# Recurrence kernel: the fourth level of an inverse in one piece, and two pieces of filling work swapped

## The chip, the cores and the metric

The kernel runs on one core of a Trainium2 chip. The metric is the device time in microseconds of one execution. A profiled execution has a span as well, from its first instruction to its last.

## What is computed

Three parts follow one another. The first is a recurrence over 768 steps for 4 x 8 heads, each with a 40 x 40 state:

```
y[t]  = r[t] . state
Sa    = state . a[t]
state = state * w[t] - outer(Sa, b[t]) + outer(v[t], k[t])
```

The second part is a mixture of four attention experts over the heads' outputs (scores, softmax, top 2 of 4), the third a gated MLP with a mixing over the sequence. The change touches the first part alone, which takes about the first half of the time.

## The kernel before, in words

The recurrence is computed in blocks of 128 steps. One block of one batch entry, with all its 8 heads, is a *unit*; there are 4 x 6 = 24. A unit has 4 chunks of 32 steps, 0 to 3. Within a chunk the steps depend on one another through a lower triangular matrix n; its inverse T is built by doubling, in five *levels*, numbered i = 0 to 4 (`level`, line 752): each multiplies a power of n by itself and by the product so far. So the "second level" is i = 1, the "fourth" i = 3 and the "fifth" i = 4. A level works on 8 blocks and issues 16 matmuls, 2 for each block; the profile counts each as two, so a whole level is 32 weight loads and 32 matmuls, two of its blocks 8 of each. After a level VectorE turns the new power (line 1059) and adds the product (line 1094, semaphore `q_added`), and ScalarE spreads the turned power over two masked copies (line 541, `spread`) and copies the power as a right operand (`copy_power`, `power_copied`; it shows as "ACT pq L533"). The next level waits for both.

The state goes from chunk to chunk through a chain of three *hops* on TensorE (`hop`, line 923) with VectorE in between (`chain`, line 1138):

- hop 0: akz times the values (line 941, needs no state) and a_ch times state_z (line 947) give g; VectorE copies it (line 1145).
- hop 1: tz times g (line 957); VectorE makes the values vu_tok in two instructions (line 1153).
- hop 2: keys times values (line 969), the state's products; VectorE adds them to the state (state_sum, line 1161) and spreads the decayed sum as state_z (line 1173), for which hop 0 of the next chunk waits.

The order of all work is written out by hand. On each engine a loop over u calls, after every hop (c, j) of chunk c, a function `between(u, c, j)` with filling work for other units (TensorE's is at line 846). Its unit numbers are t = u + 2, v = u + 1, w = u - 1 and x = u - 2. What stands in `between(u, c, 1)` runs while VectorE makes the values of the chunk, and ahead of hop 2; what stands in `between(u, c, 2)` runs behind the state's products, while VectorE makes state_sum and state_z. TensorE executes in this order, so a wait in front of filling work holds the next hop too.

Filling work that matters here, of TensorE: first Gram products of t (line 718); `turn_states(w)` (line 701) and `turn_outputs(u - 3)` (line 806), transposes of earlier states and outputs into PSUM, read by ScalarE in `states_read` (line 555, tile state_n) and `outputs_taken` (line 594, tile y_raw); `from_values` (line 842), which adds the part of the outputs that comes from the values; `turn_values` (line 696), which waits for state_n; and the levels of unit v, all on line 768. Levels 1 to 4 and the turned outputs use the same PSUM bank, 3, so level 1 waits until y_raw is taken (`y_taken`). ScalarE's order in a unit begins with the two spreads of tz, then states_read, then outputs_taken. In the last two units TensorE also has matmuls that fold two weight matrices (line 747).

Of the kernel before, what the change touches and what calls it, by code (L numbers as in the profile page):

```python
# [25 lines left out]
def recurrence(nc, z, loads, weights, x_out, shared):  # L26
# [17 lines left out]
    N8 = 2 * NC  # L44
# [7 lines left out]
    with ExitStack() as ctx:  # L52
# [11 lines left out]
        def at(u, s, c=None):  # L64

            return u * per[s] + (per[s] if c is None else c)
# [97 lines left out]
        kb_read = sem("kb_read", 2)  # L164
# [9 lines left out]
        vu_read = sem("vu_read", 2)  # L174
# [54 lines left out]
        def valid(u):  # L229
            return 0 <= u < UNITS  # L230
# [300 lines left out]
        def _(act):  # L531
            def copy(dst, src):
                return act.activation(dst, src, ACT.Copy)  # L533

            def spread_power(u, i):

                act.wait_ge(turned[i], at(u, turned[i]))
                if u > 0:
                    act.wait_ge(level_ready[i], at(u - 1, level_ready[i]))
                for j in range(2):  # L540
                    act.activation(powers_z[:, i, :, j, :], powers[:, i, :, :], ACT.Copy, scale=parity[:, j:j + 1])\  # L541
                        .then_inc(spread[i], 1)
# [51 lines left out]
            def outputs_taken(w):  # L594

                act.wait_ge(y_turned, at(w, y_turned))
                if w > 0:
                    act.wait_ge(y_done, at(w - 1, y_done))
                copy(y_raw[0:CHANNELS, :], bank[Y_TURN_BANK][0:CHANNELS, :]).then_inc(y_taken, 1)
# [51 lines left out]
            for u in range(UNITS + 3):  # L651
                r, t, v, w, x = u + 3, u + 2, u + 1, u - 1, u - 2
                if valid(u):
                    spread_t(u)
                if u == 0:
                    copy_power(1, 0)
                    spread_power(1, 1)
                if valid(w):
                    states_read(w)
                if valid(u - 3):  # L660
                    outputs_taken(u - 3)
                if u == 0:
                    pad_a(2)
                if valid(t):
                    spread_power(t, 0)
                if valid(v):
                    spread_power(v, 2)
                    copy_power(v, 1)
                if valid(w):
                    values_read(w)  # L670
                if valid(x):
                    outputs_copied(x)
                if valid(v):
                    spread_power(v, 3)
                    copy_power(v, 2)
                if u == UNITS - 1:
                    folded(0)
                if u == UNITS:
                    folded(2)
                if valid(r):  # L680
                    pad_a(r)
                if valid(v):
                    spread_power(v, 4)
                    keys_read(v)
                if valid(t):
                    copy_power(t, 0)
                    spread_power(t, 1)
                if u == UNITS - 1:
                    folded(1)
                if u == UNITS:  # L690
                    folded(3)

        @block.tensor
        def _(pe):
# [78 lines left out]
            def turn_states(w):  # L773

                pe.wait_ge(state_done, at(w, state_done, NC - 1))
                for c in range(NC):
                    for b in range(2):
                        col = (c % 2 * 2 + b) * P
                        ins = turn_channels(bank[TURN_BANKS[c // 2]][:, col:col + P],
                                            state[:, w % 2, c, b].rearrange("p a d -> p (a d)"))  # L780
                ins.then_inc(state_turned, 1)
# [19 lines left out]
            def turn_outputs(w):  # L801

                pe.wait_ge(y_copied, at(w, y_copied))
                for c in range(NC):
                    src = y_tok[:, c, :, :].rearrange("p x d -> p (x d)")
                    ins = pe.transpose(bank[Y_TURN_BANK][0:CHANNELS, c * P:c * P + P], src[:, 0:CHANNELS], ident[:, :])
                ins.then_inc(y_turned, 1)
# [27 lines left out]
            def from_values(w, first):  # L835

                for c in range(first, first + 2):
                    for x in range(2):
                        for q in range(Q):
                            a, p, g, blk = place(c, q)  # L840
                            col = c * X + x * D
                            pe.matmul(bank[Y_BANK][rows32(g), col:col + D], rvu[rows64(p), c * 2 + x, 1 - a, :],
                                      kb_tok[rows64(p), w % 3, a, c, x, :], start=False, stop=(c < 2),
                                      skip_group_check=True)

            def between(u, c, j):


                t, v, w, x = u + 2, u + 1, u - 1, u - 2
                if (c, j) == ((0, 0) if u > 0 else (0, 2)) and valid(t):  # L850
                    first_grams(t)
                if (c, j) == (0, 0):
                    if valid(w):
                        if valid(v - 1):
                            pe.wait_ge(kb_read, at(v - 1, kb_read))
                        else:
                            pe.wait_ge(vu_read, at(w - 1, vu_read))
                        turn_states(w)
                    if valid(u - 3):

                        if valid(u):
                            pe.wait_ge(q_added[4], at(u, q_added[4]))
                        else:
                            pe.wait_ge(oi_read, 2)
                            pe.wait_ge(y_taken, at(u - 4, y_taken))
                        turn_outputs(u - 3)
                if (c, j) == (0, 1):
                    if valid(x):
                        from_values(x, 2)
                    if valid(v):  # L870
                        if valid(u - 3):
                            pe.wait_ge(y_taken, at(u - 3, y_taken))
                        level(v, 1, 0, 2)
                if (c, j) == (0, 2) and valid(v):
                    level(v, 1, 2, N8)
                if (c, j) == (1, 0):
                    if valid(w):
                        pe.wait_ge(state_n_read, at(w, state_n_read))
                        turn_values(w)
                    if valid(x):  # L880
                        from_states(x, 2)
                if (c, j) == (1, 1):
                    if valid(t):
                        level(t, 0, 0, 4)
                    if valid(v):
                        level(v, 2, 0, 2)
                if (c, j) == (1, 2) and valid(v):
                    level(v, 2, 2, N8)
                if (c, j) == (2, 0):
                    if valid(t):  # L890
                        grams(t, 1)
                    if valid(w):
                        if valid(x):
                            pe.wait_ge(y_copied, at(x, y_copied))
                        r_products(w)
                if (c, j) == (2, 1):
                    if valid(t):
                        pe.wait_ge(akz_read, at(t, akz_read))
                        level(t, 0, 4, N8)
                    if valid(v):  # L900
                        level(v, 3, 0, 2)
                if (c, j) == (2, 2) and valid(v):
                    level(v, 3, 2, N8)
                if (c, j) == (3, 0):
                    if valid(v):
                        if valid(w):
                            pe.wait_ge(vu_read, at(w, vu_read))
                        turn_keys(v)
                    if valid(w):
                        pe.wait_ge(rvu_read, at(w, rvu_read))  # L910
                        pe.wait_ge(state_n_read, at(w, state_n_read))
                        from_states(w, 0)
                if (c, j) == (3, 1):
                    if valid(w):
                        from_values(w, 0)
                    if valid(v):
                        level(v, 4, 0, 2)
                if (c, j) == (3, 2) and valid(v):
                    level(v, 4, 2, N8)
                for f in range(folds_upto(u, c, j) - folds_after.get((u, c, j), 0), folds_upto(u, c, j)):  # L920
                    fold(f)
# [1056 lines left out]
```

## Time and profile before

| | us |
|---|---|
| median of 3 runs | 989.86 |
| lowest and highest | 985.64, 992.79 |
| the profiled execution | 986.91 |
| its span | 985.0 |
| TensorE busy (share of the span) | 937.3 (95%) |
| TensorE weight loads busy | 676.4 (69%) |
| VectorE busy | 490.3 (50%) |
| ScalarE busy | 447.5 (45%) |

Busy time of an engine is the union of its instructions' times. TensorE appears twice, as PE (matmuls) and PEld (weight loads), which overlap; matmuls are pipelined, so starts of successive weight loads tell more of its pace than durations do. "Idle before <- X" is the idle time of the engine just ahead of an instruction and what ended it; "issue" is a wait for nothing that the profile shows.

### The profile page before, as it was taken

Reading aid. Unit: us, or ns where it says so; the run is one execution under the profiler, and the core shown is the slowest. Engines: PE = TensorE matmul, PEld = TensorE weight load, DVE = VectorE, ACT = ScalarE, POOL = GpSimd, SP = SyncE. Lnnn points to the kernel's source line nnn. Section 1 sums busy time; section 2 is a strip of 40 time slices with the busy share of each in tenths; the row PEclk is TensorE's granted clock in tenths of the full one; section 3 lists DMA queues with packets and bytes.
Section 4 is the critical chain, followed back from the end, with each engine's and each line's share of the span. In section 5 each row is a group of like instructions: output and inputs, shape, how many; then the busy total and the mean of one; then the engine's idle time right before and its main releaser. Section 6 shows DMA issues by size and latency. Waiting matters only on the chain.

```text
span 985.0 us, 36043 instructions
## 1 busy us (share of the span) xinstructions
PE 937.3 (95%) x15444; PEld 676.4 (69%) x15444; DVE 490.3 (50%) x1395; ACT 447.5 (45%) x1074; POOL 266.2 (27%) x442
## 2 busy tenths in 40 slices
PE   6899999999999999999998999999999999999998
PEld 4788888888888888886655655566555665556555
DVE  7687777677677777754155244321444214342120
ACT  6455655555555555553237234342343423434501
POOL 7444545445445545522300001100011000110021
PEclk8799999999999999999999999999999999999999
DMA  4234333335333333241160000001000000000001
GB/s 153 71 108 115 111 100 105 100 93 152 101 99 106 100 94 112 68 122 31 51 217 1 2 0 1 1 28 54 0 1 2 27 14 0 1 2 27 14 0 41
DMA packets 37455, 59.68 MB, mean 61 GB/s; under 512 B 9136, under 2 KB 24304, under 8 KB 37296
## 3 DMA queue, kind: packets, MB, share of 16 engines
q1 hardware_dynamic: 37296, 57.37, 19.6%
q8 instruction: 123, 2.02, 0.9%
q14 instruction: 36, 0.29, 0.1%
HBM read 49.49 MB, written 7.86 MB: 58 GB/s over the span
## 4 chain that ended last, share of the span: by engine, by line
PE 80%; DVE 8%; issue 6%; ACT 5%; DMA 1%; POOL 0%; DVEq 0%; ACTq 0%; POOLq 0%
PE banks L1640 13%; PE banks L768 8%; PE banks L1579 5%; PE banks L1557 5%; PE banks L1591 4%; PE banks L1531 4%; PE banks L1608 4%; PE banks L1621 4%; PE banks L701 4%; PE banks L1652 4%; PE banks L947 3%; PE banks L829 3%; PE banks L969 3%; PE banks L696 2%; DVE state_z L1173 2%
## 5 line engine op out<-in xcount | busy, mean ns | idle before, releaser
L541 ACT ACTIVATE powers_z<-powers,parity 128x256 f32<-128x256 f32 x240 | 108.5, 500 | 162.3 <-DVE powers L1059 162.1
L1428 POOL TENSOR_TENSOR v_st<-v_st,u_t 128x384 f32<-128x384 f32 x32 | 31.9, 997 | 450.5 <-DVE v_st L1795 450.5
L768 PE MATMUL banks<-pq,powers_z 64*64 64x64 f32 (+1 forms) x3072 | 132.1, 225 | 18.4 <-ACT pq L533 13.6
L1640 PE MATMUL banks<-w_st,v_n 128*128 128x384 f32 x384 | 139.0, 497 | 0.2 <-DVE v_n L1785 0.2
L768 PEld LDWEIGHTS banks<-pq,powers_z 64*64 64x64 f32 x3072 | 112.8, 138 | 25.6 <-ACT powers_z L541 17.4
L1433 ACT ACTIVATE probs_t<-banks 128x512 f32<-128x512 f32 (+1 forms) x96 | 51.7, 542 | 121.2 <-PE banks L1579 121.2
L1640 PEld LDWEIGHTS banks<-w_st,v_n 128*128 128x128 f32 x384 | 67.6, 190 | 48.1 <-issue 10.8
L480 POOL TENSOR_TENSOR state<-state_sum,dc 128x160 f32<-128x160 f32 x92 | 56.9, 619 | 106.0 <-DVE state_sum L1161 106.0
L1738 DVE CUSTOM_DVE_ANT_0 probs<-banks,hide 128x128 f32<-128x128 f32 (+5 forms) x96 | 56.0, 622 | 51.6 <-PE banks L1557 51.1
L1153 DVE SCALAR_TENSOR_TENSOR vu_tok<-banks,minus,vz_tok 128x80 f32<-128x80 f32 x192 | 48.8, 296 | 64.0 <-PE banks L957 63.0
L1447 ACT ACTIVATE probs<-probs,neg_max 128x128 f32<-128x128 f32 (+5 forms) x96 | 63.2, 660 | 31.3 <-DVE neg_max L1738 31.3
L427 POOL TENSOR_TENSOR kb_ch<-w_all,s_ch 128x512 f32<-128x512 f32 x46 | 66.1, 1439 | 37.6 <-issue 34.0
L1760 DVE TENSOR_TENSOR o_t<-banks,share_t 128x256 f32<-128x256 f32 x24 | 10.2, 425 | 100.3 <-ACT share_t L1433 88.5
L1652 PE MATMUL banks<-w,v_st 128*128 128x320 f32 x192 | 57.6, 435 | 0.0
L1579 PE MATMUL banks<-ident,probs 128*128 128x128 f32 x336 | 53.8, 281 | 1.4 <-ACT probs_t L1433 1.4
L1579 PEld LDWEIGHTS banks<-ident,probs 128*128 128x128 f32 x336 | 38.0, 140 | 23.4 <-issue 15.7
L1161 DVE TENSOR_TENSOR state_sum<-banks,state 128x160 f32<-128x160 f32 x96 | 30.6, 319 | 41.8 <-PE banks L969 41.8
L1557 PE MATMUL banks<-k_t,q_t 64*128 64x512 f32 (+3 forms) x256 | 49.1, 482 | 1.3 <-DVE k_t L1826 1.1
L1591 PEld LDWEIGHTS banks<-probs_t,vg 128*64 128x64 f32 x672 | 35.7, 136 | 20.8 <-issue 17.4
L1591 PE MATMUL banks<-probs_t,vg 128*64 128x128 f32 x672 | 47.3, 280 | 0.3 <-DVE o_t L1760 0.3
L1795 DVE TENSOR_TENSOR v_st<-banks,bias 128x384 f32<-128x384 f32 x32 | 17.8, 556 | 59.7 <-PE banks L1640 59.7
L1173 DVE TENSOR_TENSOR state_z<-state_sum,dc_side 128x320 f32<-128x320 f32 x92 | 45.3, 493 | 3.2
(168 smaller groups left out, 1770.0 us busy)
## 6 DMA issues: line engine op xcount, KB each, us to landing
w_all<-decays_dram SPq DMA_DIRECT2D x48, 160.0 KB
w_all<-kb_ch_dram SPq DMA_DIRECT2D x48, 160.0 KB
vz_tok<-vz_tok_dram SPq DMA_DIRECT2D x24, 320.0 KB, 3.2
rz_ch<-rz_ch_dram SPq DMA_DIRECT2D x48, 160.0 KB
a_raw<-a_ch_dram SPq DMA_DIRECT2D x48, 80.0 KB
vc_tok<-vc_tok_dram SPq DMA_DIRECT2D x24, 160.0 KB, 2.7
x_dram<-y_ch SPq DMA_DIRECT2D x48, 80.0 KB
out_dram<-out_tok SPq DMA_DIRECT2D x24, 160.0 KB, 1.8
```

Source lines behind the costliest of these rows:

```text
L427: pool.tensor_tensor(*keys_by_decays(u, a), ALU.mult).then_inc(kb_scaled, 1)
L480: pool.tensor_tensor(state[:, v % 2, d, :, :, 0:D], state_sum[:, :, :].rearrange("p (a b) d -> p b a d", b=2), dc[:, v % 4, d].rearrange(" ...
L541: act.activation(powers_z[:, i, :, j, :], powers[:, i, :, :], ACT.Copy, scale=parity[:, j:j + 1])\
L768: ins = pe.matmul(to[r, k * n:k * n + n], powers_z[r, i, k, :, :].rearrange("p j t -> p (j t)"), right, start=True, stop=True)
L1173: dve.tensor_tensor(to_z, state_sum[:, :, :].unsqueeze(2).to_broadcast([P, Q, 2, D]), dc_side[:, v % 4, d].unsqueeze(3).to_broadcast([P, Q ...
L1447: act.activation(probs[:, s % 3, a, 0:width], probs[:, s % 3, a, 0:width], ACT.Exp, scale=-1.0, bias=neg_max[:, i, e:e + 1], accum_out=den ...
L1557: ins = pe.matmul(bank[2 * a + (j if width > 512 else s % 2)][:, 0:w], q_t[rows, p, i * P:i * P + P], k_t[rows, p, c:c + w], start=True, s ...
L1579: ins = pe.transpose(turn_bank(n, m)[:, x * P:x * P + P], src, ident[:, :])
L1591: ins = pe.matmul(bank[O_BANK][64 * a:64 * a + HD, p * P:p * P + P], vg[:, j, e * HD:e * HD + HD], probs_t[:, s % 2, a * (i + 1) + j, :], ...
L1640: ins = pe.matmul(bank[M_BANK + j % 2][:, 0:TH], v_n[:, i, d * P:d * P + P], w_st[:, i, t], start=(i == 0), stop=(i == BLOCKS - 1))
L1652: ins = pe.matmul(bank[M_BANK + i % 2][:, 0:F], gated[:, d, i * P:i * P + P], w_2[:, d, :], start=(d == 0), stop=(d == DT - 1))
L1738: dve.tensor_tensor_reduce(out=probs[:, s % 3, a, 0:width], in0=both[:, 0:width], in1=hide[:, S - width:S], scale=-1.0, scalar=3e38, op0=A ...
```

## The change

On TensorE three things move. The fourth level, which was split into two blocks in `between(u, 2, 1)` and six in `between(u, 2, 2)`, is issued in one piece in `between(u, 2, 2)`, with its wait. `turn_outputs` goes ahead of `turn_states` in `between(u, 0, 0)`, and ScalarE's `outputs_taken` ahead of `states_read` to match. In `between(u, 0, 1)` and `between(u, 3, 1)` the first two blocks of the second and of the fifth level go ahead of `from_values`. No operation is added or removed.

```diff
@@ ScalarE, the loop over u @@
+                if valid(u - 3):
+                    outputs_taken(u - 3)
                 if valid(w):
                     states_read(w)
-                if valid(u - 3):
-                    outputs_taken(u - 3)
@@ TensorE, between @@
                 if (c, j) == (0, 0):
+                    if valid(u - 3):
+
+                        if valid(u):
+                            pe.wait_ge(q_added[4], at(u, q_added[4]))
+                        else:
+                            pe.wait_ge(oi_read, 2)
+                            pe.wait_ge(y_taken, at(u - 4, y_taken))
+                        turn_outputs(u - 3)
                     if valid(w):
...
                         turn_states(w)
-                    if valid(u - 3):
...
-                        turn_outputs(u - 3)
                 if (c, j) == (0, 1):
-                    if valid(x):
-                        from_values(x, 2)
                     if valid(v):
                         if valid(u - 3):
                             pe.wait_ge(y_taken, at(u - 3, y_taken))
                         level(v, 1, 0, 2)
+                    if valid(x):
+                        from_values(x, 2)
...
                         level(t, 0, 4, N8)
-                    if valid(v):
-                        level(v, 3, 0, 2)
                 if (c, j) == (2, 2) and valid(v):
-                    level(v, 3, 2, N8)
+
+                    level(v, 3)
...
                 if (c, j) == (3, 1):
+                    if valid(v):
+                        level(v, 4, 0, 2)
                     if valid(w):
                         from_values(w, 0)
-                    if valid(v):
-                        level(v, 4, 0, 2)
```

## Rows read from the trace of the kernel before

**Rows 1.** busy time by stretch, the recurrence. Stretch; busy us (instructions) of each engine; clock

```profile
50.00:440.00 390.00, 366.42 (x11374) 323.12 (x11372) 279.81 (x778) 223.03 (x528) 191.13 (x306) 1.00 0.37 106
```

**Rows 2.** waits of TensorE, whole execution. Waited for; total us, times, longest

```profile
PE banks L768 <- ACT pq L533: 13.6, 22, 1.3
...
PEld banks L768 <- ACT powers_z L541: 18.4, 25, 1.4
...
PEld banks L947 <- DVE state_z L1173: 12.1, 71, 0.3
...
PEld banks L768 <- ACT y_raw L533: 4.1, 17, 0.2
```

**Rows 3.** timeline, unit 9, chunk 2. Start, length, engine, line, tiles, count [idle before]

```profile
208.33 0.51 DVE L1153 SCALAR_TENSOR_TENSOR vu_tok<-banks,minus,vz_tok 128x80 f32<-128x80 f32 x2
...
208.83 0.36 ACT L533 ACTIVATE pq<-banks 128x256 f32<-128x256 f32 x1
...
209.30 0.30 PEld L768 LDWEIGHTS banks<-pq,powers_z 64*64 64x64 f32 x7 [0.67 <-ACT powers_z L541]
...
209.48 0.11 PEld L969 LDWEIGHTS banks<-vu_tok,kb_tok 64*40 64x40 f32 x1
...
210.40 0.36 PEld L941 LDWEIGHTS banks<-vc_tok,akz 64*64 64x64 f32 x8
...
210.92 0.16 PEld L947 LDWEIGHTS banks<-state_z,a_ch 128*32 128x32 f32 x8 [0.16 <-DVE state_z L1173]
```

**Rows 4.** timeline, unit 9, chunk 1

```profile
204.66 0.29 PEld L969 LDWEIGHTS banks<-vu_tok,kb_tok 64*40 64x40 f32 x16
...
204.84 0.80 PEld L768 LDWEIGHTS banks<-pq,powers_z 64*64 64x64 f32 x24
...
205.15 0.33 DVE L1161 TENSOR_TENSOR state_sum<-banks,state 128x160 f32<-128x160 f32 x1 [0.60 <-PE banks L969]
...
205.55 0.33 PEld L941 LDWEIGHTS banks<-vc_tok,akz 64*64 64x64 f32 x8
```

**Rows 5.** timeline, unit 14, chunk 2

```profile
301.15 0.36 ACT L533 ACTIVATE pq<-banks 128x256 f32<-128x256 f32 x1
...
301.51 0.51 DVE L1153 SCALAR_TENSOR_TENSOR vu_tok<-banks,minus,vz_tok 128x80 f32<-128x80 f32 x2 [0.90 <-PE banks L957]
...
303.52 0.16 PEld L947 LDWEIGHTS banks<-state_z,a_ch 128*32 128x32 f32 x8 [0.16 <-DVE state_z L1173]
```

**Rows 6.** timeline, unit 9, chunk 3

```profile
211.97 0.91 ACT L541 ACTIVATE powers_z<-powers,parity 128x256 f32<-128x256 f32 x2 [1.61 <-DVE powers L1059]
...
212.66 0.31 PEld L957 LDWEIGHTS banks<-g_tok,tz 64*64 64x64 f32 x8
...
213.13 0.51 DVE L1153 SCALAR_TENSOR_TENSOR vu_tok<-banks,minus,vz_tok 128x80 f32<-128x80 f32 x2 [0.89 <-PE banks L957]
...
213.76 0.41 PEld L969 LDWEIGHTS banks<-vu_tok,kb_tok 64*40 64x40 f32 x16
```

**Rows 7.** timeline, unit 11, chunk 0

```profile
235.75 0.44 PEld L806 LDWEIGHTS banks<-ident,y_tok 128*104 128x104 f32 x4
...
236.37 0.31 PEld L957 LDWEIGHTS banks<-g_tok,tz 64*64 64x64 f32 x8 [0.18 <-issue]
...
236.69 0.60 ACT L533 ACTIVATE y_raw<-banks 104x512 f32<-104x512 f32 x1
...
236.85 0.51 DVE L1153 SCALAR_TENSOR_TENSOR vu_tok<-banks,minus,vz_tok 128x80 f32<-128x80 f32 x2 [0.71 <-PE banks L957]
...
237.72 0.45 DVE L1059 STREAM_TRANSPOSE powers<-n_t 128x256 f32<-128x256 f32 x1
...
238.09 0.29 DVE L1161 TENSOR_TENSOR state_sum<-banks,state 128x160 f32<-128x160 f32 x1
```

**Rows 8.** timeline of weight loads behind the last unit

```profile
481.21 0.37 PEld L842 LDWEIGHTS banks<-kb_tok,rvu 64*32 64x32 f32 x32 [0.76 <-issue]
481.63 0.40 PEld L806 LDWEIGHTS banks<-ident,y_tok 128*104 128x104 f32 x4
```

More of the change, by code:

```diff
@@ L852, in between @@
                 if (c, j) == (0, 0):
[L853 to L858, printed above, removed]
                     if valid(u - 3):
@@ L866, in between @@
                         turn_outputs(u - 3)
+                    if valid(w):
+                        if valid(v - 1):
+                            pe.wait_ge(kb_read, at(v - 1, kb_read))
+                        else:
+                            pe.wait_ge(vu_read, at(w - 1, vu_read))
+                        turn_states(w)
                 if (c, j) == (0, 1):
-                    if valid(x):
-                        from_values(x, 2)
                     if valid(v):
```

## The prediction

> **What bounds the kernel now.** I began with busy time by stretch. In the stage of the recurrence TensorE is busy 366.42 of 390.00 us at a granted clock of 1.00 [rows 1], and the change touches this stage alone; the clock is at its 2.4 GHz level throughout, so the clock plays no part. TensorE is nearly full, so an idle gap of TensorE counts, but only if no other chain covers it. The waits of TensorE over the whole execution come next: matmuls of the levels waited 22 times for a copy of pq by ScalarE, 13.6 us; their weight loads waited 18.4 us for the spreads of powers_z; 17 short waits for y_raw make 4.1 us; the weight loads that take state_z waited 71 times, 12.1 us [rows 2]. The first two are one wait, at the start of the fourth level (i = 3), once a unit. The last shows where VectorE's chain (sum, then state_z) ends later than TensorE's filling work.
>
> **Chunk 2 of a unit, where the gain would be.** I read it in the timeline [rows 3]. The values vu_tok are ready at 208.33 + 0.51 = 208.84. The copy of pq ends at 208.83 + 0.36 = 209.19, and the fourth level's first weight load starts 0.11 later, at 209.30. The state's products (line 969), queued behind it, start at 209.48, 0.64 after their values; in the next chunk they start 0.12 after them (213.13 + 0.51 = 213.64, then 213.76) [rows 6]. So 0.52 us are lost in chunk 2. They can't all be had back. Now 8 + 16 + 24 loads stand between 209.30 and the first load of line 941 at 210.40; those of line 941 end at 210.76, and line 947, which needs state_z, starts at 210.92 [rows 3].
>
> **Fourth level in one piece behind the state's products.** Removed: 8 loads and matmuls (two blocks) ahead of line 969, with the wait. Added: the same 8 behind it. Step by step, in the times of rows 3:
> - Line 969 starts 0.12 after the values, at 208.96. Its 16 loads need about 0.18: in chunk 1 they start at 204.66 and the level's at 204.84 [rows 4]. Done at 209.14.
> - The level still can't start before 209.30, since its copy ends when it did; only a wait of 0.16 is left, with the level behind it and no longer line 969.
> - The level's 32 loads: 24 take 204.84 to 205.55 = 0.71 [rows 4], so 0.0296 each and 0.95 for 32. Line 941 starts at 210.25.
> - Line 941 takes 0.33 [rows 4], to 210.58. The change from half-height weights to full-height ones costs 0.05 where nothing else holds it (481.21 + 0.37 = 481.58, then 481.63 [rows 8]). Line 947 could start at 210.63.
> - VectorE's chain would allow it earlier: in unit 14 the copy was early (301.15 + 0.36 = 301.51), so no wait stood ahead of line 969, and line 947 started 1.50 after the values (301.51 + 0.51 = 302.02, then 303.52) [rows 5]. That is 208.84 + 1.50 = 210.34. TensorE is the later of the two, with 210.63.
>
> Gain: 210.92 - 210.63 = 0.29 a unit. So of 0.52 lost, what comes back is about the time of line 969's own loads, now done inside the wait, plus the small slack (0.11) that state_z had over TensorE. The bounds: 0 if line 947 can't start earlier at all, 0.58 (210.92 - 210.34) if the level met no wait and cost TensorE nothing.
>
> It counts in 21 units: 23 units prepare a following one, and in two of them a stall earlier in the chunk left the copy ready (unit 14 of [rows 5] is one); the 22 waits of [rows 2] are these 21 and one ahead of the first unit. In those, line 969 was not late, and the 8 loads behind it lengthen TensorE's part: 8 x 0.0296 = 0.24 less the slack of 0.11, +0.13 each. Sum: -21 x 0.29 + 2 x 0.13 = -5.8 us.
>
> Line 969 is weighed against a rule. The rows show 16 loads in 0.29 us, the last of which takes about 0.11 [rows 3, 4], so they start some 12 ns apart. The Trainium skill, "TensorE: Matmul & The Clock Gate", section "Wait — 56ns, not 53.3ns?", says that starts of small matmuls are never closer than about 25 ns. By that, the products would take an estimated 16 x 25 = 0.40 us, end at 209.36 and so cover the whole wait, line 947 would start at 210.69, and the change would give -21 x 0.23 + 0.3 = -4.5 us. The trace disagrees, and I go by the rows; the verdict would be the same.
>
> **Outputs turned ahead of states.** On TensorE (chunk 0, first step) line 806's 4 transposes and line 701's 8 swap places; both still stand between the Gram products and line 957. The pause of 0.18 behind line 806 (235.75 + 0.44 = 236.19, then 236.37) [rows 7] will follow the other kind. It could vanish or double: 0.18 either way, and I take 0. turn_outputs carries its waits along, for t_t of this unit and for y_tok; both are long fulfilled where it stands now, and still behind the Gram products, as t_t is made ahead of the g_tok copy of this chunk; what queues behind them is line 701 and then line 957. On ScalarE y_raw goes ahead of state_n, which comes up to its 0.60 later. state_n's first reader is turn_values, in the next chunk, thus after the sum of 238.09; state_n now ends about where y_raw starts, 236.69 [rows 7], so even 0.60 later it is 0.8 early. GpSimd, which reads y_raw, gets to it by its own order after the third chunk's state.
>
> **Second level ahead of the outputs from values (chunk 0).** The wait for y_raw goes. Today the level starts behind y_raw's end (236.69 + 0.60 = 237.29), just about when the values are ready (236.85 + 0.51 = 237.36) [rows 7]; the products behind it lose under 0.1. Yet VectorE is the bound here: after the values it makes n_t and turns it (237.72 to 238.17), and the sum starts only when that is nearly over, at 238.09, while products that start 0.12 after their values would allow 237.48 + 0.49 = 237.97 (0.49 from line 969 to the sum: 204.66 to 205.15 [rows 4]). Worth 0; the transpose hides it, and without that cover it would be 0.12 a unit at most.
>
> **Fifth level ahead of the outputs from values (chunk 3).** Here a wait is put ahead of covered work. The spreads end at 211.97 + 0.91 = 212.88, line 957's loads at 212.66 + 0.31 = 212.97 [rows 6]; with 0.11 from end to load the level may start at 212.99. It and the 32 loads of line 842 take 0.33 (7 loads in 0.30 [rows 3] and one more start of 0.03) and 0.37 [rows 8], to 213.69, and line 969 waits for its values until 213.76 anyway. All of it keeps its distance to line 947 of this chunk, so a shift of chunk 2 moves it as a whole. Cost 0, with only 0.07 to spare; if each change between tile shapes costs 0.05 more, still 0.
>
> **Sum.** 985.0 - 5.8 = 979.2 for the span, 981.1 for the profiled execution (986.9). That one is 0.3% under the median of the runs, 989.86; on the median the change gives **984.1 us**.
>
> **Rivals.**
> - *The wait disappears* (15%). Were the copy early enough, as in unit 14, the level would follow at 209.14, line 947 at 210.47: 0.45 a unit, 9.5 us in all, 9.2 with the two units, near 980.7. Against it: ScalarE's spreads and copy keep their length, and what releases them lies in the same chunk.
> - *Nothing comes back* (15%). If TensorE were full in the sense that any order takes equally long, or line 941 or 947 were held by what no row shows, the time stays: 990, give or take 1. For it: TensorE's 94% busy. Against it: the wait at 208.84 to 209.30 is true idle time.
> - *The fifth level holds the state* (5%, slower). Its place is chunk 3, line 768 ahead of line 842, for the spread of turned powers. Price: every 0.1 us by which ScalarE is later than 212.88 delays line 969 by as much, once past the 0.07 spare; 0.5 us late would be 0.43 x 22 = +9.5 less 5.8, about 994. It decides from some 0.33 us late, where it eats the whole gain. Against it: ScalarE stands idle for 1.61 us before those spreads and starts them on VectorE's turn [rows 6], which keeps its place behind line 947.
>
> **How the numbers follow.** The forecast has 65%: 0.29 +- 0.1 a unit, 982 to 987. With the rivals on both sides and the spread of the runs (985.6 to 992.8, so a median can sit 2 or 3 us off), 8 in 10 lie in 978 to 990. About 1% is what a measurement can tell from no change here, thus 980.0 and 999.8 as borders. Faster by over 1%: half of the first rival, and of the forecast what a low median would bring, 0.17. Slower by over 1%: the last rival at its far end, 0.04. Within 1%: 0.79.
>
> **What would show it.** In the trace after: line 969 of chunk 2 starts about 0.12 after vu_tok; the wait of line 768 for pq shrinks from 0.6 to about 0.16 and stands behind line 969; line 947 of chunk 3 starts some 1.79 after the values, without a wait for state_z (so those waits fall from 71 by some 20); the waits for y_raw are gone with no change in chunk 0's length; chunk 3 keeps its length. Chunk 2 shorter by 0.3 and all others as long as before confirm the sum. If line 947 there starts 1.50 after the values, the first rival holds; if chunk 3 is longer, the last.

## The result, and the profile after

The changed kernel takes 986.4 us in the median of 20 runs, the kernel before 991.2 in 20 runs beside them. The ratio is 0.9956, with a 95% interval of 0.9937 to 0.9975, so 2.5 to 6.2 us less: faster, and by less than 1%. The prediction was 5.8 us less. A second timing of the changed kernel, in other rounds, gave 0.9958 (0.9939 to 0.9977).

The waits of TensorE first, over the whole execution (waited for; total us, times, longest). They answer to [rows 2]:

```profile
PE banks L768 <- ACT pq L533: 1.5, 2, 0.8
...
PEld banks L946 <- DVE state_z L1172: 11.2, 54, 0.9
...
PEld banks L768 <- ACT powers_z L541: 2.9, 3, 1.4
...
PEld banks L968 <- issue: 12.4, 31, 0.8
```

The wait for pq was 13.6 us in 22 places and is 1.5 in 2. Part of that idle time only has another end: TensorE's weight loads stood idle ahead of line 969 (968 here), with no semaphore named, for 5.3 us in 9 places before and for 12.4 in 31 now, mostly in chunk 2, where they now wait for the values. The weight loads waited 71 times for state_z and do so 54 times now: in chunk 2 TensorE comes to that point after VectorE. No wait of TensorE for y_raw is listed any more.

Chunk 2 of unit 9 in the timeline answers to [rows 3]. Lines 941, 947, 957, 969, 1153 and 1161 of before are 940, 946, 956, 968, 1152 and 1160 here.

```profile
210.71 0.51 DVE L1152 SCALAR_TENSOR_TENSOR vu_tok<-banks,minus,vz_tok 128x80 f32<-128x80 f32 x2
...
211.20 0.36 ACT L533 ACTIVATE pq<-banks 128x256 f32<-128x256 f32 x1
...
211.33 0.29 PEld L968 LDWEIGHTS banks<-vu_tok,kb_tok 64*40 64x40 f32 x16 [0.33 <-issue]
...
211.68 1.04 PEld L768 LDWEIGHTS banks<-pq,powers_z 64*64 64x64 f32 x32
...
211.81 0.32 DVE L1160 TENSOR_TENSOR state_sum<-banks,state 128x160 f32<-128x160 f32 x1
...
212.17 0.49 DVE L1172 TENSOR_TENSOR state_z<-state_sum,dc_side 128x320 f32<-128x320 f32 x1
...
212.61 0.35 PEld L940 LDWEIGHTS banks<-vc_tok,akz 64*64 64x64 f32 x8
...
213.00 0.16 PEld L946 LDWEIGHTS banks<-state_z,a_ch 128*32 128x32 f32 x8
```

The values are ready at 210.71 + 0.51 = 211.22 and line 968 follows at 211.33. The copy of pq ends at 211.56, the level starts 0.12 later at 211.68, and 32 loads later, at 212.61, line 940 begins. Line 946 starts at 213.00 with no idle time before it, 1.78 after the values (2.08 before; 1.79 was predicted). VectorE's sum starts at 211.81, 0.59 after the values, and state_z is done at 212.66, before line 946 asks for it. TensorE has become the bound of this chunk.

To see all units I took the distance from the first load of line 947 in one chunk to that in the next, over units 4 to 20, which are 17. The table has the lower quartile as the usual value. In chunks 1 and 3 most units lie within 0.01 us of it (11 to 16 of the 17), in chunk 2 7 to 15 do, and in chunk 0 only 5 to 8; the others are longer. "Stalls" is the sum of all that lies above the usual values, whatever its cause, and "at 1.2 GHz" the part of it in chunks in which the granted clock was at its lower level for a while. "Stretch" is the time from unit 4 to unit 21: 17 usual units plus the stalls, to within 0.4 us.

| kernel (one profile each) | chunk 0 | 1 | 2 | 3 | unit | stalls | at 1.2 GHz | stretch |
|---|---|---|---|---|---|---|---|---|
| before | 4.62 | 4.38 | 4.87 | 4.23 | 18.10 | 5.8 | 0 | 313.2 |
| changed | 4.60 | 4.38 | 4.57 | 4.22 | 17.78 | 6.3 | 0 | 308.5 |
| changed, second profile | 4.60 | 4.38 | 4.57 | 4.22 | 17.78 | 8.3 | 0 | 310.4 |
| e1 fourth level only | 4.62 | 4.39 | 4.57 | 4.23 | 17.81 | 10.3 | 1.6 | 312.8 |
| e2 swaps only | 4.60 | 4.39 | 4.87 | 4.23 | 18.09 | 5.7 | 0 | 312.9 |
| e3 wait ahead | 4.60 | 4.39 | 4.71 | 4.22 | 17.93 | 10.5 | 5.6 | 315.2 |
| e4 turns only | 4.60 | 4.39 | 4.87 | 4.23 | 18.08 | 4.2 | 0 | 311.4 |
| e5 Gram products behind | 4.46 | 4.38 | 4.57 | 4.22 | 17.63 | 14.0 | 3.1 | 313.5 |
| e6 power first | 4.60 (lowest) | 4.38 | 4.41 | 4.22 | 17.62 | 11.7 | 0 | 311.3 |
| e12 power first, timed | 4.60 | 4.38 | 4.41 | 4.22 | 17.63 | 11.5 | 2.9 | 311.0 |
| e7 both | 4.46 | 4.39 | 4.41 | 4.22 | 17.48 | 15.9 | 0 | 312.7 |

Unit 22 is outside the table, and there the change gave three times as much. Its chunk 2 takes 5.16 us before and 4.24 now; e2 and e4, which keep the level split, have 5.17 and 5.16, and e1, which has only the level moved, 4.24. A matmul that folds weights (line 747; its row counts two loads) stands in this chunk behind the level's first two blocks and ahead of line 969. Before:

```profile
448.31 0.51 DVE L1153 SCALAR_TENSOR_TENSOR vu_tok<-banks,minus,vz_tok 128x80 f32<-128x80 f32 x2 [0.52 <-PE banks L957]
...
448.81 0.34 PEld L768 LDWEIGHTS banks<-pq,powers_z 64*64 64x64 f32 x8 [0.67 <-ACT powers_z L541]
...
449.22 0.30 PEld L747 LDWEIGHTS banks<-w_all 128*128 128x128 f32 x2
450.27 0.26 PEld L969 LDWEIGHTS banks<-vu_tok,kb_tok 64*40 64x40 f32 x16 [0.76 <-issue]
```

and after:

```profile
447.19 0.30 PEld L747 LDWEIGHTS banks<-w_all 128*128 128x128 f32 x2
...
447.31 0.51 DVE L1152 SCALAR_TENSOR_TENSOR vu_tok<-banks,minus,vz_tok 128x80 f32<-128x80 f32 x2 [0.52 <-PE banks L956]
...
448.25 0.26 PEld L968 LDWEIGHTS banks<-vu_tok,kb_tok 64*40 64x40 f32 x16 [0.76 <-issue]
```

The wait held the folding matmul, and that held line 969, which started 1.45 after the values (448.82) and now starts 0.43 after them (447.82).

The profiled spans alone would mislead: 985.0 and 984.6. The stretch is 4.7 shorter, but unit 4 began 3.7 later, and 0.6 went behind unit 21. The start tells why, in busy time by stretch (the last three numbers are granted clock, DMA share and GB/s), before and after:

```profile
0.00:60.00 60.00, 46.61 (x1000) 37.11 (x1002) 44.18 (x98) 32.37 (x63) 34.28 (x84) 0.83 0.35 110
```

```profile
0.00:60.00 60.00, 48.92 (x860) 39.57 (x860) 39.65 (x87) 30.49 (x58) 31.30 (x79) 0.66 0.31 98
```

A mean of 0.83 between the levels of 2.4 and 1.2 GHz means the lower one for a third of the 60 us, 0.66 for two thirds. The second profile of the same changed kernel has 0.86 there, so the lower clock at the start does not come with the change.

### The profile page after: what moved, and what is told of

Its sections match the earlier page's. It is cut to its first block, busy times and chain, and to the rows that moved or that the text cites. A ratio compares the mean times of both kernels' runs of the same rounds, so it can differ in the third digit from the quotient of the medians.

```text
span 984.6 us, 36043 instructions
## 1 busy us (share of the span) xinstructions
PE 946.3 (96%) x15444; PEld 685.4 (70%) x15444; DVE 490.4 (50%) x1395; ACT 450.4 (46%) x1074; POOL 265.8 (27%) x442
## 3 DMA queue, kind: packets, MB, share of 16 engines
q8 instruction: 123, 2.02, 0.9%
## 4 chain that ended last, share of the span: by engine, by line
PE 85%; DVE 9%; issue 3%; ACT 2%; DMA 1%; DVEq 0%; POOL 0%; ACTq 0%; POOLq 0%
PE banks L1639 13%; PE banks L768 7%; PE banks L1578 5%; PE banks L1556 5%; PE banks L1590 4%; PE banks L1530 4%; PE banks L1607 4%; PE banks L1620 4%; PE banks L1651 4%; PE banks L701 4%; PE banks L956 4%; PE banks L968 3%; PE banks L946 3%; PE banks L829 3%; DVE state_z L1172 3%
## 5 line engine op out<-in xcount | busy, mean ns | idle before, releaser
L541 ACT ACTIVATE powers_z<-powers,parity 128x256 f32<-128x256 f32 x240 | 108.6, 500 | 157.2 <-DVE powers L1058 157.0
L968 PE MATMUL banks<-vu_tok,kb_tok 64*40 64x40 f32 x1536 | 39.1, 210 | 7.9 <-DVE vu_tok L1152 6.7
```

Of the source, the lines that this page charges most:

```text
L968: ins = pe.matmul(bank[S_BANK + q % 2][rows40(x), a * D:a * D + D], kb_tok[rows64(p), u % 3, a, c, x, :], vu_tok[rows64(p), u % 2, c, x, a ...
```

## The experiments

**e1, e2: the two halves of the change.** e1 has the fourth level alone:

```diff
-                    if valid(v):
-                        level(v, 3, 0, 2)
                 if (c, j) == (2, 2) and valid(v):
-                    level(v, 3, 2, N8)
+                    level(v, 3)
```

> The kernel before with one part of the change: the fourth level in one piece behind the state's products. My theory: chunk 2, from line 947 to the next line 947, goes from 4.87 to 4.57 us as in the changed kernel (line 969 0.115 after the values, the level starting 0.34 to 0.35 after the end of line 969's wait, line 947 without a wait for state_z); chunks 0, 1 and 3 stay at 4.61, 4.38 and 4.22. In time: 5.5 to 6.5 us faster than before, ratio about 0.994. Rival (the gain needs the swaps too, since each only clears the way for the next wait): chunk 2 above 4.65 us, ratio above 0.997.

Measured: chunk 2 at 4.57, the others as before; ratio 0.9965 (0.9935 to 0.9996). The chunk lengths are those of the theory to 0.01 us, and the rival's 4.65 is out. The ratio misses the narrow 0.994 by less than its own interval, which also covers nearly no change: about 3.5 us, where the theory said 5.5 to 6.5.

e2 is the changed kernel with those lines as they were before.

> The changed kernel with the fourth level split again, two blocks with the wait ahead of the state's products: only the swaps are left (outputs turned first, second and fifth level ahead of the outputs from values). My theory: chunk 2 stays at 4.87 us, chunk 0 goes from 4.615 to 4.60, chunk 3 stays at 4.22; in time 0 to 0.5 us faster, ratio 1.000 within its interval. Rival (clearing the y_raw wait of 0.24 us in 17 units counts): chunk 0 at 4.40 us, 4 us faster, ratio 0.996. Rival (the fifth level ahead holds the state): chunk 3 above 4.30 us.

Measured: chunks at 4.60, 4.39, 4.87, 4.23, as the theory had them, and neither rival's 4.40 or 4.30. Yet the ratio is 0.9971 (0.9944 to 0.9999), about 3 us faster, where the chunks say 0.3. The interval nearly reaches 1; what the swaps may give beyond the chunk lengths no profile here places.

**e3: is it the wait or the eight loads?** The changed kernel, with the level's waits ahead of line 969 and all its work behind:

```diff
                         level(t, 0, 4, N8)
+                    if valid(v):
+                        pe.wait_ge(spread[3], at(v, spread[3]))
+                        pe.wait_ge(power_copied[2], at(v, power_copied[2]))
                 if (c, j) == (2, 2) and valid(v):
                     level(v, 3)
```

> The changed kernel, but TensorE waits for spread and copy of the fourth level ahead of the state's products (where the level's first two blocks stood), while all 8 blocks of the level stay behind them. It tells what costs: the wait, or the 8 loads in front. My theory: TensorE has 16 + 32 loads of work behind the wait whatever their order, and it is the bound, so nothing is left of the gain of chunk 2: line 969 starts 0.46 after the values, in place of 0.63, the sum 0.17 earlier, but line 947 starts 2.02 to 2.08 after the values: chunk 2 at 4.82 to 4.87 us. Rival (VectorE's chain is the bound, so what is ahead of line 969 alone counts): chunk 2 at 4.70 us or less.

Measured: 4.71, between the two. Unit 11, chunk 2 (line 969 is 971 here, 941 is 943, 947 is 949):

```profile
249.98 0.51 DVE L1155 SCALAR_TENSOR_TENSOR vu_tok<-banks,minus,vz_tok 128x80 f32<-128x80 f32 x2
250.40 0.36 ACT L533 ACTIVATE pq<-banks 128x256 f32<-128x256 f32 x1
...
250.83 0.29 PEld L971 LDWEIGHTS banks<-vu_tok,kb_tok 64*40 64x40 f32 x16 [0.55 <-ACT powers_z L541]
...
251.01 1.04 PEld L768 LDWEIGHTS banks<-pq,powers_z 64*64 64x64 f32 x32
...
251.67 0.49 DVE L1175 TENSOR_TENSOR state_z<-state_sum,dc_side 128x320 f32<-128x320 f32 x1
...
251.94 0.35 PEld L943 LDWEIGHTS banks<-vc_tok,akz 64*64 64x64 f32 x8
...
252.33 0.16 PEld L949 LDWEIGHTS banks<-state_z,a_ch 128*32 128x32 f32 x8
```

The values are ready at 250.49. Line 971 starts at 250.83, 0.07 after the copy's end (250.76) and not 0.11. The level's 32 loads follow at 251.01, line 943 at 251.94 and line 949 at 252.33, with no idle time and not held by state_z (251.67 + 0.49 = 252.16): TensorE is the bound here too. (In most units the copy ends later against the values, and the same steps come 0.42 and 1.92 after them, where 0.46 and 2.02 to 2.08 were expected.) My expectation forgot a term that the prediction had: before, line 947 was held by state_z, TensorE having 0.11 to spare. So the 0.30 of chunk 2 has two parts: 0.16 for getting the eight loads out from ahead of the state's products (VectorE's chain is no longer the late one, 0.11, and the wait alone ends 0.04 sooner), and 0.14 for putting the wait itself behind them.

**e4: turned outputs first, alone.** The kernel before with `turn_outputs` ahead of `turn_states`, and `outputs_taken` ahead of `states_read`.

> The kernel before with only the turned outputs ahead of the turned states, on TensorE and ScalarE. My theory: from line 947 to line 957 of chunk 0 it is 2.024 us before and 2.01 here (the pause after the last transpose is shorter by 0.01 to 0.02 when the last one has 104 columns instead of 128); the wait of line 768 for y_raw in chunk 0 is gone, line 969 starts 0.115 after the values in place of 0.154, and the sum doesn't move, 0.73 to 0.74 after the values, since VectorE's turn of n_t ends there. Rival (the pause moves with the order and doubles): 2.10 or more.

Measured: from line 947 to 957 in chunk 0 it takes 2.014 (2.025 before), line 969 starts 0.116 after the values, and the sum 0.734 after them, exactly as before. All three as expected: the wait for y_raw was there and cost nothing.

**e6: is the wait that is left on the path?** The changed kernel with VectorE's order in chunk 2 turned round:

```diff
                 if (c, j) == (2, 0):
-                    if valid(t):
-                        keys_of_a(t)
                     if valid(v):
                         level_read(v, 2)
+                    if valid(t):
+                        keys_of_a(t)
```

> The changed kernel, but in chunk 2 VectorE turns the power of the third level before it makes akz from the Gram products, so ScalarE has the copy of pq some 0.7 us earlier and the fourth level finds no wait behind the state's products. It tells whether the 0.16 us of wait left there is on the path. My theory (TensorE's path from the wait over 32 loads, line 941 and line 947 sets the end of chunk 2): line 947 starts 1.61 to 1.63 after the values in place of 1.78, chunk 2 at 4.40 to 4.42 us in place of 4.57. Rival (line 947 is held by something else, or the first level's second half, which waits for akz, now holds the products): chunk 2 at 4.55 or more.

Measured: chunk 2 at 4.41. Unit 18, chunk 2:

```profile
370.08 0.36 ACT L533 ACTIVATE pq<-banks 128x256 f32<-128x256 f32 x1
...
370.48 0.51 DVE L1152 SCALAR_TENSOR_TENSOR vu_tok<-banks,minus,vz_tok 128x80 f32<-128x80 f32 x2 [0.34 <-PE banks L956]
...
371.10 0.29 PEld L968 LDWEIGHTS banks<-vu_tok,kb_tok 64*40 64x40 f32 x16 [0.33 <-issue]
...
371.28 1.04 PEld L768 LDWEIGHTS banks<-pq,powers_z 64*64 64x64 f32 x32
...
372.21 0.35 PEld L940 LDWEIGHTS banks<-vc_tok,akz 64*64 64x64 f32 x8
...
372.61 0.16 PEld L946 LDWEIGHTS banks<-state_z,a_ch 128*32 128x32 f32 x8
```

The copy of pq is over at 370.44, long before the values (370.99). The level follows line 968 at 371.28 with no gap, and line 946 starts 1.62 after the values. The 0.16 was on the path, as the first rival of the prediction had it: 0.45 a unit by its sum, and 4.87 - 4.41 = 0.46 here, are to be had when the copy is early. One profile and one time, 980.9 us.

**e5, e7: the same idea in chunk 0.** The changed kernel with the first Gram products in `between(u, 0, 1)` and the second level in one piece behind the state's products; e7 has this and the edit of e6.

```diff
-                if (c, j) == ((0, 0) if u > 0 else (0, 2)) and valid(t):
+                if (c, j) == ((0, 1) if u > 0 else (0, 2)) and valid(t):
                     first_grams(t)
...
-                        level(v, 1, 0, 2)
+                        if u == 0:
+                            level(v, 1, 0, 2)
                     if valid(x):
                         from_values(x, 2)
                 if (c, j) == (0, 2) and valid(v):
-                    level(v, 1, 2, N8)
+                    level(v, 1, 2 if u == 0 else 0, N8)
```

> The changed kernel, with filling work of chunk 0 moved for the same reason that moved the fourth level: the first Gram products (line 718, 32 loads) go from ahead of line 957 to behind it, ahead of the outputs from values, and the second level is issued in one piece behind the state's products. My theory: from line 947 to 957 of chunk 0 TensorE is the bound, so this falls from 2.01 to about 1.58 us; the products start about 0.25 after the values in place of 0.115, hidden by VectorE's turn of n_t; line 947 comes 1.75 after the values in place of 1.60, since TensorE carries 8 more loads. Chunk 0 from 4.60 to about 4.32 us, the others unchanged. Rival (VectorE's n_t now waits for the Gram products and holds the sum): chunk 0 at 4.55 us or more.

> Both of the two edits together, Gram products behind line 957 in chunk 0 and the power turned first in chunk 2, as a version that should beat both kernels. By my theory the gains add: chunk 0 at 4.32, chunk 2 at 4.41, so 0.44 us a unit, over 20 units some 9 us less than the changed kernel; against before about 13 to 14 us less, ratio 0.986. Rival (stalls of instruction issue and VectorE take back half): ratio 0.991 or more.

> The changed kernel once more, in the same rounds as the version above, and for a second profile of it. Chunk medians as in the first profile (4.60, 4.38, 4.57, 4.22 us); ratio to before 0.993 to 0.997. What differs between the two profiles is the stalls of issue and the stretches at the 1.2 GHz clock at the start, which are not the change's: I expect each to differ by 1 to 3 us between two profiles of one kernel.

Measured: e5 has chunk 0 at 4.46, half the gain expected. Unit 13, chunk 0 (line numbers as before):

```profile
273.29 0.31 PEld L957 LDWEIGHTS banks<-g_tok,tz 64*64 64x64 f32 x8
...
273.64 0.49 PEld L718 LDWEIGHTS banks<-az_ch,kb_ch 128*32 128x32 f32 x32
...
273.76 0.51 DVE L1153 SCALAR_TENSOR_TENSOR vu_tok<-banks,minus,vz_tok 128x80 f32<-128x80 f32 x2 [0.32 <-PE banks L957]
274.23 0.37 PEld L842 LDWEIGHTS banks<-kb_tok,rvu 64*32 64x32 f32 x32
...
274.37 0.42 DVE L1067 TENSOR_TENSOR n_t<-banks,upper 128x256 f32<-128x256 f32 x1
274.65 0.26 PEld L969 LDWEIGHTS banks<-vu_tok,kb_tok 64*40 64x40 f32 x16
...
275.20 0.28 DVE L1161 TENSOR_TENSOR state_sum<-banks,state 128x160 f32<-128x160 f32 x1
...
276.12 0.16 PEld L947 LDWEIGHTS banks<-state_z,a_ch 128*32 128x32 f32 x8
```

The stretch to line 957 fell by 0.39 as hoped. But the values are ready at 274.27, n_t starts only at 274.37 because it now waits for the Gram products, and line 842, pushed behind them, ends at 274.60, so that line 969 starts 0.38 after the values; the sum is at 0.93 in place of 0.73. So 4.46 lies between the theory (4.32) and the rival (4.55), with the rival's mechanism at work. And the stalls went up to 14.0 us in e5, of which 3.1 at the lower clock, and 15.9 in e7: e7 has the shortest unit of all and a ratio of only 0.9925 (0.9901 to 0.9950), where 0.986 was expected. The changed kernel beside it (e8) gave 0.9958, its chunks unchanged; its stalls differ by 2.0 us and its first hop by 2.6 us from the first profile.

**e9, e10, e11: are the stalls a matter of how many instructions TensorE draws?**

```diff
-                    if valid(t):
-                        level(t, 0, 0, 4)
...
                         pe.wait_ge(akz_read, at(t, akz_read))
-                        level(t, 0, 4, N8)
+                        pe.wait_ge(spread[0], at(t, spread[0]))
+                        level(t, 0, N8 - 1, N8)
```

> The kernel before with 7 of 8 blocks of the first level left out, ahead of the state's products of chunks 1 and 2, where TensorE has idle time anyway: 56 weight loads and matmuls fewer a unit (5%), part of the computation not done. It tells whether the stalls of issue, each of which ends 2.2 to 2.9 us after a 16 KB instruction packet began, come from how densely TensorE draws instructions. My theory (instruction supply): chunk lengths without a stall stay at 4.61, 4.38, 4.87, 4.22 us, and the time above them, 5.8 us over 17 units before, falls below 4; ratio to before 0.996 to 0.999. Rival (the stalls are fixed spots of the program or come from the data transfers beside them): the sum stays at 5 us or more.

> The changed kernel with the same 7 of 8 blocks of the first level left out. My theory (instruction supply): chunks without a stall at 4.60, 4.38, 4.57, 4.22; the time above them, 6.3 and 8.3 us in two profiles of the full kernel, falls below 5, and the change is worth 6 us (ratio to the thinned kernel before 0.994), the whole of what the chunk lengths say. Rival (stalls independent of the number of instructions): 6 to 8 us of stalls stay.

> The version with Gram products behind line 957 and the power turned first, with the same 7 of 8 blocks of the first level left out. Chunks without a stall at 4.46, 4.38, 4.41, 4.22, 0.61 us a unit less than before. My theory: the 15.9 us of stalls over 17 units of the full version fall below 10, and the kernel is 8 to 12 us faster than the thinned kernel before, ratio to before near 0.985. Rival: stalls stay at 14 us or more and the ratio to before stays at 0.992.

All three leave out 7 of the 8 blocks of the first level, so a part of the inverse is not computed.

Measured, as stalls over 17 units and ratio to before: e9 2.9 us, 1.0016 (0.9985 to 1.0046); e10 8.9 us, 0.9940 (0.9915 to 0.9965); e11 18.3 us, 0.9963 (0.9930 to 0.9995). Usual chunks moved by 0.02 at most. Of e11's 18.3, 7.2 lie in three chunks of units 17 and 18 at the lower clock, which leaves 11.1 against 15.9 in e7. So the stalls fell in e9 and, the clock taken off, in e11, though not below the 10 expected; in e10 they were to fall below 5, and stand at 8.9 against 6.3 and 8.3. Each is one profile, and not of a typical execution: e9's was the fastest of its twelve (986.7, with a median of 995.3), e11's one of the slowest (992.8, median 990.2). In time, e9 is no faster than before and e11 no faster than e7; e10 against the thinned kernel before is 0.9940 / 1.0016 = 0.992, near the 0.994 expected. That the number of instructions sets the stalls is not shown, and these three runs don't rule it out either.

**e12: the better version, timed.** The kernel of e6.

> The version with the power turned first in chunk 2, timed. Its one look gave 980.9 us with chunk 2 at 4.41 and chunk 0 unchanged at 4.60 us where no stall lies in it. By the chunk lengths it is 0.47 us a unit shorter than before, 20 units, 9.4 us: ratio 0.990 to 0.992 if the gain is kept, and 3 us less than the changed kernel. Rival (what is won behind a removed wait is given back to stalls of issue, as in the version with both edits, 0.9925 for 0.61 us a unit): ratio 0.993 to 0.996.

Measured: 981.4 us in the median, ratio 0.9896 (0.9861 to 0.9931), 11 us less than before and some 6 less than the changed kernel. It beats both. The ratio is just under the 0.990 to 0.992 expected. A little of it may be the clock: its six runs have a mean granted clock of 0.986, the eleven of before beside them 0.984, and over the 76 runs of before in the rounds of these experiments 0.001 more of mean clock goes with 0.6 us less (a fit), which makes an estimate of 1 to 2 us.

## Why the prediction was right

**The bound and the place.** That an idle gap of TensorE counts only where nothing else covers it was borne out in both directions: the gap in chunk 2 counted, the one at y_raw in chunk 0 didn't (e4).

**The fourth level.** Predicted 0.29 a unit, measured 0.30, in e1 alone as well; line 947 1.79 after the values, measured 1.78. The terms hold one by one in the rows above: line 969 after 0.11 to 0.12, the level 0.12 after the copy, 0.93 for 32 loads (0.95), no wait for state_z behind. The 16 loads of line 968 take 0.29 to the end of the last, and line 946 came at 1.78. By the rule of the Trainium skill, "TensorE: Matmul & The Clock Gate", section "Wait — 56ns, not 53.3ns?", that starts of small matmuls are never closer than about 25 ns, an estimate of 1.85 would follow; the trace disagrees, and the prediction was right to go by the rows. That the full 0.52 of idle time would not come back is the point; e3 shows how the 0.30 splits, e6 that 0.16 more was held by the copy. The cost where the copy was early was right as well: in unit 14, line 947 came 1.50 after the values before and 1.62 now, and chunk 2 went from 5.15 to 5.27, +0.12 where +0.13 was predicted, with the same stall in both profiles.

**The count.** 21 units had the wait, as predicted, though not as the prediction read it: of the 22 waits of [rows 2] two stand ahead of the first unit, and that of unit 17 is not among them. One of the 21 is unit 22, which gave 0.92 and not 0.29: the prediction had only the 8 loads behind the wait there, not the folding matmul. That price was too low by 0.6 us in all.

**The three costs at nothing.** Turned outputs: 0.01 us a unit, from 2.025 to 2.014. Second level ahead: the products come 0.04 sooner and the sum not at all. Chunk 0 of unit 14:

```profile
291.78 0.60 ACT L533 ACTIVATE y_raw<-banks 104x512 f32<-104x512 f32 x1 [0.18 <-PE banks L806]
...
292.39 0.31 PEld L956 LDWEIGHTS banks<-g_tok,tz 64*64 64x64 f32 x8
...
292.62 0.32 PEld L768 LDWEIGHTS banks<-pq,powers_z 64*64 64x64 f32 x8
...
292.87 0.51 DVE L1152 SCALAR_TENSOR_TENSOR vu_tok<-banks,minus,vz_tok 128x80 f32<-128x80 f32 x2 [0.71 <-PE banks L956]
...
293.50 0.26 PEld L968 LDWEIGHTS banks<-vu_tok,kb_tok 64*40 64x40 f32 x14
...
293.74 0.45 DVE L1058 STREAM_TRANSPOSE powers<-n_t 128x256 f32<-128x256 f32 x1
294.11 0.28 DVE L1160 TENSOR_TENSOR state_sum<-banks,state 128x160 f32<-128x160 f32 x1
```

The values are ready at 293.38, line 968 follows at 293.50, and the sum at 294.11 stands behind the turn of n_t, which began at 293.74; 0.73 after the values, as before. y_raw ends at 292.38, ahead of the second level, whose first load is at 292.62; no wait is left there, with 0.24 to spare.

Fifth level ahead: chunk 3 stays at 4.22, here in unit 14, answering to [rows 6]:

```profile
305.68 0.91 ACT L541 ACTIVATE powers_z<-powers,parity 128x256 f32<-128x256 f32 x2 [2.01 <-DVE powers L1058]
...
306.37 0.31 PEld L956 LDWEIGHTS banks<-g_tok,tz 64*64 64x64 f32 x8
...
306.64 0.31 PEld L768 LDWEIGHTS banks<-pq,powers_z 64*64 64x64 f32 x8
...
306.85 0.51 DVE L1152 SCALAR_TENSOR_TENSOR vu_tok<-banks,minus,vz_tok 128x80 f32<-128x80 f32 x2 [0.89 <-PE banks L956]
306.99 0.37 PEld L842 LDWEIGHTS banks<-kb_tok,rvu 64*32 64x32 f32 x32
...
307.47 0.29 PEld L968 LDWEIGHTS banks<-vu_tok,kb_tok 64*40 64x40 f32 x16
```

The spreads end at 306.59, the level starts at 306.64 (0.05 later, not 0.11), behind it line 842 ends at 307.36, and line 968 starts at 307.47, 0.11 after its values (307.36). The spare of 0.07 was enough, and the condition of the slower rival, spreads that end late, was not met. Its chance was not worked out well: 0.04 for slower by over 1% needs a time over 999.8, and the rival's own price, at 0.5 us late, was 994.

**The sum.** By the chunks, 20 units at 0.30, 0.92 for unit 22, 0.12 less for unit 14 and 0.3 for chunk 0 make 7.1 us. The timings say 4.4 and 4.2, and their intervals reach from 2.3 to 6.2. So the mechanism and the gain of each unit are shown, but some 3 us of them are missing in the time, more than the intervals allow. That the forecast of 5.8 stands so near the measured 4.4 is in part luck: the price of unit 22 was too low, and something outside the sum took more than that back. A candidate is the stalls, 6.3 and 8.3 us in the changed kernel against 5.8 before; others are the clock at the start and whatever lies outside units 4 to 20. None is shown, since two profiles of one kernel differ by as much, and e2 errs the other way, 3 us faster where its chunks say 0.3.

**What to carry over.** Filling work that carries a wait belongs behind the critical work of its slot, and what comes back is not the wait but the lesser of two slacks: that of the other engine's chain, and that of the engine itself with the filler behind. Once a wait has moved behind, look at what feeds it (here VectorE's order) before looking for more filler to move. Look also for the units in which other work queues behind the same wait, as in unit 22. A gain read from typical units must be checked against stalls that are in no typical unit.

## What the runs showed of the hardware

**Stalls of issue go with instruction packets.** In the profiles of before and after, between 85 and 440 us, every idle time of TensorE over 0.33 us that no semaphore explains (18 of them, those ahead of line 969 left out, where the values can be what is waited for) ended 2.3 to 3.0 us after a 16 KB packet of the instruction queue had begun, though such packets come only every 4.2 us (83 and 84 in this time). In all fourteen profiles there are 149 such idle times, those ahead of line 957 left out as well, and 148 of them ended 2.2 to 3.6 us after a packet had begun. That the engine waits for its instructions is the likely reading; no run takes the packets away to show it. One of them, in the weight loads of the changed kernel:

```profile
180.88 0.53 PEld L718 LDWEIGHTS banks<-az_ch,kb_ch 128*32 128x32 f32 x32
...
182.38 0.40 PEld L806 LDWEIGHTS banks<-ident,y_tok 128*104 128x104 f32 x4 [0.97 <-issue]
```

It stands idle for 0.97 us up to 182.38, and the only instruction packet in the 3 us to 182.5 (queue, kind: packets, MB, share) is

```profile
q8 instruction: 1, 0.02, 2.6%
```

Over the eleven profiles of the table, with the chunks at 1.2 GHz taken off, the stalls grow as the usual unit shrinks: 4.2 to 5.8 us at 18.1 us a unit, 4.9 to 11.7 between 17.6 and 17.9, and 15.9 at 17.48. Why they grow stays open; that the usual unit does not tell the time is seen in e7, 0.15 us a unit shorter than e12, with a ratio of 0.9925 to its 0.9896.

**The lower clock came behind long stalls.** In five of the fourteen profiles (e1, e3, e5, e11, e12) the granted clock fell to 0.50, the 1.2 GHz level, within units 4 to 20, and each time TensorE had stood idle for 0.9 to 2.1 us of issue shortly ahead. In e3:

```profile
360.22 0.25 PEld L959 LDWEIGHTS banks<-g_tok,tz 64*64 64x64 f32 x6 [1.69 <-issue]
```

```profile
362.20:372.20 10.00, 10.00 (x197) 8.96 (x193) 4.66 (x12) 3.75 (x9) 2.72 (x6) 0.50 0.24 65
```

The three chunks that this touches are 5.6 us longer than usual, the stall included. Not every stall does it: 1.26 us up to 219.24 in the kernel before left the clock at 1.00.

**The clock at the start differs between executions.** In the first 60 us the mean granted clock was 0.83 before, 0.66 and 0.86 in two profiles of one changed kernel; the first hop began at 29.7, 32.4 and 29.8 us. The two profiles of the changed kernel are of one program, so this difference is none of a change. By unit 4, which began at 108.6 and 102.1 us in them, it had grown to 6.5 us, about twice the difference of their spans (984.6 and 981.5); so single profiles are compared by the stretch, not by the span.
